# A fused attention kernel on one core: the order of masked copies, reciprocals and value products in its first stage

## The reference

```python
# batch 4, heads 8, seq 576, head_dim 64; window = 128
scores = (q @ k.T) / 8 + slope[h] * -(i - j)
scores = where((i - j >= 0) & (i - j < window), scores, -1e9)
attn = exp(scores - max); attn /= attn.sum(-1) + 1e-9
x = (attn @ v)                       # heads side by side: batch x 576 x 512
h = relu(x @ w_in)                   # 512 -> 1024, halves u and v
v_s = w_spatial @ layernorm(v) + b_spatial
x = (u * v_s) @ w_out
# then: gate, top 2 of 4 experts, causal attention per expert, sum
```

## Time and profile before

| | us |
|---|---|
| three runs: median (lowest to highest) | 489.86 (488.61 to 491.36) |
| the profiled execution | 489.27 |
| its span, from the first to the last instruction | 487.4 |
| busy in it: TensorE / its weight loads | 475.3 / 408.5 |
| busy in it: VectorE / ScalarE / GpSimd | 317.8 / 272.9 / 202.9 |

### The profile page before, as it was taken

The page is one execution under the profiler, slowest core; times in us unless marked ns, Lnnn a source line. Parts: engine busy times, 40 slices in busy tenths (PEclk is TensorE's granted clock), DMA queues, the critical chain, the costliest instruction groups (busy, mean ns, idle before and its releaser), DMA issues.

```text
span 487.4 us, 10761 instructions
## 1 busy us (share of the span) xinstructions
PE 475.3 (98%) x3858; PEld 408.5 (84%) x3858; DVE 317.8 (65%) x1247; ACT 272.9 (56%) x827; POOL 202.9 (42%) x373
## 2 busy tenths in 40 slices
PE   8799999999999999999999999999999999999996
PEld 5577998999776789999876689999877679999974
DVE  7886775367778855337778855436777875235783
ACT  6776572346676644245766745334776663335663
POOL 4361614523434418742244525760343443461431
PEclk9899999999999999999999999999999999999999
DMA  7919420004110081002311073002301000000111
GB/s 230 326 64 245 179 86 1 1 1 135 46 33 23 13 240 42 1 0 53 107 34 44 1 196 98 1 1 48 101 32 56 0 1 2 2 1 12 38 45 54
DMA packets 33512, 31.64 MB, mean 65 GB/s; under 512 B 6002, under 2 KB 24434, under 8 KB 33460
## 3 DMA queue, kind: packets, MB, share of 16 engines
q1 hardware_dynamic: 33460, 30.97, 21.2%
HBM read 23.88 MB, written 4.72 MB: 59 GB/s over the span
## 4 chain that ended last, share of the span: by engine, by line
PE 66%; DVE 17%; ACT 11%; issue 4%; POOL 1%; DVEq 0%
PE bank L1412 14%; PE bank L1414 14%; PE bank L1413 14%; ACT p L830 7%; PE bank L1399 5%; PE bank L1483 5%; DVE ring L943 4%; PE bank L1441 3%; DVE p L1194 2%; PE bank L1690 2%; PE bank L1668 2%; PE bank L1418 2%; DVE ring L954 2%; PE bank L1419 1%; DVE pt L1030 1%
## 5 line engine op out<-in xcount | busy, mean ns | idle before, releaser
L539 POOL TENSOR_SCALAR ring<-ring,r 128x128 f32<-128x128 f32 x144 | 60.2, 430 | 86.1 <-DVE r L963 85.8
L625 POOL TENSOR_SCALAR p<-p,r,wgt 128x128 f32<-128x128 f32 (+3 forms) x64 | 38.3, 610 | 93.3 <-DVE wgt_last L1241 50.0
L653 ACT ACTIVATE ring<-ring,neg 128x128 f32<-128x128 f32 x144 | 56.7, 396 | 21.3 <-DVE ring L954 18.1
L830 ACT ACTIVATE p<-p,neg 128x128 f32<-128x128 f32 (+4 forms) x72 | 41.6, 579 | 29.6 <-DVE neg L1194 29.6
L943 DVE CUSTOM_DVE_ANT_0 ring<-bank,bias 128x256 f32<-128x256 f32 (+1 forms) x128 | 43.5, 384 | 2.3 <-PE bank L1399 2.0
L589 POOL TENSOR_TENSOR g_lo<-uT,g_hi 128x288 fp32r<-128x288 f32 x32 | 25.2, 814 | 36.4 <-ACT g_hi L796 20.4
L1412 PE MATMUL bank<-g_hi,w_c_hi 128*128 128x288 f32 x128 | 38.6, 301 | 0.2
L1412 PE MATMUL bank<-x_hi,w_in_hi 128*128 128x288 f32 x128 | 38.2, 298 | 0.0
L1412 PE MATMUL bank<-w_spatial_hi,vn_hi 128*128 128x288 f32 x128 | 37.8, 295 | 0.0
L1414 PE MATMUL bank<-x_hi,w_in_lo 128*128 128x288 f32 x128 | 37.7, 295 | 0.0
L1414 PE MATMUL bank<-w_spatial_hi,vn_lo 128*128 128x288 f32 x128 | 37.7, 294 | 0.0
(11 more groups left out here) (193 smaller groups left out, 1449.0 us busy)
## 6 DMA issues: line engine op xcount, KB each, us to landing
v_in<-v SPq DMA_DIRECT2D x16, 256.0 KB, 4.0
out<-o_sb SPq DMA_DIRECT2D x16, 256.0 KB, 2.0
q<-qT SPq DMA_DIRECT2D x15, 256.0 KB, 4.6
k<-kT SPq DMA_DIRECT2D x15, 256.0 KB, 5.1
v_minus_v_of_tile_above<-v SPq DMA_DIRECT2D x9, 256.0 KB, 3.8
w_in_raw<-w_in SPq DMA_DIRECT2D x4, 512.0 KB, 6.2
w_cat_raw<-wcat SPq DMA_DIRECT2D x1, 1544.0 KB, 6.8
w_spatial_raw<-wsT SPq DMA_DIRECT2D x1, 1152.0 KB, 9.3
```

The costliest lines, as they stand in the source:

```text
L539: last = nc.gpsimd.tensor_scalar(p, p, r1[:, i % 2, h:h + 1], 0.0, ALU.mult, ALU.add)
L625: nc.gpsimd.tensor_scalar(p, p, r3[:, i % 2, e:e + 1], by, ALU.mult, ALU.mult).then_inc(s3_sd, 1)
L653: nc.scalar.activation(x, x, ACT.Exp, bias=neg1[:, u % SLOTS1:u % SLOTS1 + 1], scale=-1.0, accum_out=sum1[:, i % 2, h:h + 1]).then_inc(s1_ ...
L830: nc.scalar.activation(p, p, ACT.Exp, bias=neg3[:, w % 4:w % 4 + 1], scale=-1.0, accum_out=sum3[:, i % 2, es[0]:es[0] + 1]).then_inc(s3_ex, 1)
```

## The change

Four orders change; no instruction is added or taken away.

On TensorE, `values1(m)` issues the unmasked products of both groups, then waits for the masked copy, then issues the masked products of both. Before, it waited for the masked copy between the first group's unmasked and masked products. Since the two groups' sums are now open at once in one bank, only the first group of a tile (g % 4 == 0) starts with the flag that clears the bank.

On ScalarE, at m = 3 and 5 `copy_pt1(m)` goes ahead of both exponentials instead of between them, so that the copy of m = 3 lies between group 8 and group 9. In row 0 the splitting of `w_in` parts (1, 0) and (1, 1) goes ahead of the exponentials of group 8.

On VectorE, at m = 3 the masked copy goes from behind `join1(10)` and `reciprocal1(9)` to ahead of them, at m = 5 from behind `reciprocal1(13)` and `join1(14)` to directly behind `bias1(14)`; at m = 2 `reciprocal1(6)` and `reciprocal1(7)` each move ahead of the bias step they stood behind, at m = 0 `reciprocal1(3)` moves ahead of `join1(5)`, at m = 5 `join1(14)` moves ahead of `reciprocal1(13)`. In row 0 `low_w_in(1, 0)` and `(1, 1)` go ahead of `join1(9)`.

```diff
@@ ScalarE, row @@
                     elif m == 2:
                         copy_pt1(2)
-                        for g in (6, 7, 8):
-                            exp1(b, g)
+                        exp1(b, 6)
+                        exp1(b, 7)
+                        if first:
+                            high_w_in(1, 0)
+                            high_w_in(1, 1)
+                        exp1(b, 8)
+                    elif m in (3, 5):
+                        copy_pt1(m)
+                        exp1(b, 2 * m + 3)
+                        exp1(b, 2 * m + 4)
...
-                            if first and at[k] == m:
+                            if first and at[k] == m and m != 2:
                                 high_w_in(half, k)
@@ VectorE, row @@
                     if m == 0 and not first:
                         copy_pt1_second(0)
+                        reciprocal1(b, 3)
                         join1(b, 5)
-                        reciprocal1(b, 3)
                         reciprocal1(b, 4)
...
                     elif m == 2:
                         copy_pt1_second(2)
                         join1(b, 7)
+                        reciprocal1(b, 6)
                         bias1(b, 8)
-                        reciprocal1(b, 6)
+                        reciprocal1(b, 7)
                         bias1(b, 9)
-                        reciprocal1(b, 7)
                         join1(b, 8)
+                        if first:
+                            low_w_in(1, 0)
+                            low_w_in(1, 1)
                         join1(b, 9)
+                    elif m == 3:
+                        bias1(b, 10)
+                        reciprocal1(b, 8)
+                        copy_pt1_second(3)
+                        join1(b, 10)
+                        reciprocal1(b, 9)
+                        bias1(b, 11)
+                        join1(b, 11)
+                        reciprocal1(b, 10)
+                    elif m == 5:
+                        bias1(b, 14)
+                        copy_pt1_second(5)
+                        join1(b, 14)
+                        reciprocal1(b, 13)
+                        bias1(b, 15)
+                        join1(b, 15)
+                        reciprocal1(b, 14)
                     elif m < ND1 - 3:
                         bias1(b, 2 * m + 4)
-                        if m == 3:
-                            reciprocal1(b, 8)
-                        else:
-                            reciprocal1(b, 2 * m + 3)
+                        reciprocal1(b, 2 * m + 3)
                         join1(b, 2 * m + 4)
-                        if m == 3:
-                            reciprocal1(b, 9)
                         copy_pt1_second(m)
...
@@ TensorE, values1 @@
-                                                    values[:, h, :], pt[:, part, c:c + r], start=start, stop=stop)
+                                                    values[:, h, :], pt[:, part, c:c + r], start=start, stop=stop,
+                                                    skip_group_check=qb > 0)
...
                     for g in (2 * m, 2 * m + 1):
-                        product(g, v_in[:, qb - 1], 0, True, False)
-                        if g % 2 == 0:
-                            pe.wait_ge(s1_h2, ND1 * b + m + 1)
+                        product(g, v_in[:, qb - 1], 0, g % 4 == 0, False)
+                    pe.wait_ge(s1_h2, ND1 * b + m + 1)
+                    for g in (2 * m, 2 * m + 1):
                         if first:
                             product(g, v_in[:, qb], 1, False, False)
                         product(g, v_step[:, qb - 1], 1, False, True)
```

2 lines of the change are left out of this document (1 added, 1 removed).

## The result

The changed kernel takes 485.39 us, the median of seven runs (484.71 to 486.76); the kernel before, run beside it, 489.38 us (median of seven, 488.59 to 491.36). The ratio is 0.9925, with a 95% interval from 0.9903 to 0.9946: 0.75% faster. The profiled execution of the changed kernel is the quickest of its seven, 484.71 us with a span of 482.9 us, against 489.27 and 487.4 before.

What follows compares the result with a forecast made beforehand. TensorE, busy 98% of the span, bounds the kernel; only its first-stage waits can be won. 3.0 us for rows 1 to 3 plus 1.4 for row 0 gives 4.4, so 485.2 us, range 482.3 to 488.6.

Steps and rivals of the forecast that it cites:

- m = 0: Rows 1 to 3, group 3's reciprocal ahead of a join: rescale starts earlier, 0.2 us a row taken (bounds 0 and 0.33).
- m = 2 and 3: Rows 1 to 3: waits ahead of group 7's transposes and m = 3's masked products go; next scores 0.85 us earlier.
- what is late next?: Question asked at m = 2 and 3 once group 7's wait goes; answer: ScalarE, group 8's exponentials, whose join comes 0.2 us later.
- m = 5: Rows 1 to 3: masked copy is there before TensorE's masked products, so their wait goes, 0.33 us a row.
- The give-backs of `low_x`: Rows 1 to 3: `low_x(1)` and `low_x(2)` each end some 0.2 us after TensorE wants them, subtracted twice a row.
- Row 0: First batch row: earlier `w_in` splits start TensorE's products sooner, part lost waiting for m = 4's masked copy; 1.4 us taken.
- The reordered products: TensorE's new value product order costs nothing; bounds 0.05 us either way for each of 32 masked steps, 1.6 us in all.
- A: Rival: VectorE and ScalarE set the pace from m = 3 to 5; a row keeps 0.4 us, 487.5 us; chance 0.20 with D.
- B: Rival: rescales of groups 8 and 9 drawn out, m = 4's transposes wait 2.4 us; 492.4 us, slower; chance 0.08.
- C: Rival: no new `low_x` wait, 1.7 us a row, 2.4 in row 0; 481.8 us; within the forecast's 0.72 chance.
- D: Rival: transposes, not exponentials, hold m = 3's copy, so moving it wins nothing in rows 1 to 3; chance 0.20 with A.

Runs made afterwards that it cites:

- the corrected kernels: Changed kernel with bias 15 ahead of reciprocal 13 and the masked copy reading PSUM: 484.18 us; with row 0's `low_x(1)` behind m = 4's masked copy too: 483.62 us.

## Why the prediction was right, and where it wasn't

The forecast was 485.2 us, the measurement 485.39. The sum held, 3.0 for rows 1 to 3 against 2.76 measured and 1.4 for row 0 against 1.54. Step by step it was less right than that, and some of the closeness is luck. The schedule was that of row 1, which gained 0.81; three such rows make 2.4, and the other 0.3 is row 2's longer wait, which the schedule didn't know. And the forecast counts from 489.86 and 489.27 us, while the kernel before came out at 489.38 in seven runs: between the medians the gain is 3.99, not 4.4.

**m = 0: right.** 0.2 taken, 0.26 by the run that undoes it, and the wait that it removes is 0.24.

**m = 2 and 3: right in mechanism, 0.07 too large.** The scores of m = 4 start 1.02 us earlier against the transposes of m = 0 (13.21 instead of 14.23), where the steps say 0.2 + 0.85. With 0.24 of that from m = 0, 0.78 is left for m = 2 and 3. That the reciprocals alone would only move the wait to the copy was the reading of "what is late next?", and the run with them alone shows it: 0.76 us removed, nothing won. Alone m = 2 gives -0.08 a row, and taking m = 3 away costs 0.63. That the two need each other is argued from these; the changed kernel without the reciprocals' order of m = 2 wasn't run. What the working had too low was the masked copy, 0.69 us where 0.83 were needed, since the rescale of group 8 now runs beside it. That leaves the wait of some 0.18 us ahead of the masked products of m = 3 that was forecast to go, and of which reading PSUM takes 0.14. I had let only GpSimd suffer from that meeting; VectorE does as well. The rescale itself, 1.40 us, was allowed for and within its slack.

**m = 5: wrong.** I credited 0.33 us, because the wait for the masked copy goes. It goes, and in rows 1 and 3 the step is worth nothing: undone, the stretches are 0.05 us shorter. Only row 2 gains by it, 0.27 us. The step that failed is the question "what is late next?" for TensorE at this place. I followed the copy, the rescale of group 13 and `low_x(2)`, but not the scores of m = 8, which wait for bias 15. On VectorE that step stands behind the masked copy, join 14 and reciprocal 13 in either order, so the edit only changes which of two waits of TensorE takes the time; and it had 0.05 us of slack, as the rows above show. One look at the slack of the next instruction with a reader would have given 0.05 in place of 0.33. And the wait takes back more than the 0.33: the gap ahead of these scores grew from 0.17 to 0.66 us, by 0.49. TensorE was early by 1.02 and by 0.33, but from the transposes of m = 0 the last reading of bias 15 comes only 0.78 us earlier (21.44 instead of 22.22), and with the 0.05 of slack that is the 0.83 by which the scores of m = 8 come earlier (21.64 instead of 22.47). So the row's gain is what VectorE's chain gained, and not a sum over TensorE's waits.

**The give-backs of `low_x`: wrong.** Twice 0.2 us were taken off for `low_x(1)` and `low_x(2)`. Neither wait is there. `low_x(1)` starts at 157.20, 1.59 us after the scores of m = 4 where the working had 1.7, and it's there by 157.89, in time for the `v_product` at 157.95. The working's own figures gave a wait of 0.1 there, and I had rounded it up to 0.2; the rest is the 0.1 us by which it comes earlier after the scores than worked out. `low_x(2)` has time because the scores of m = 8 are late: it ends at 165.56, and its `v_product` stands at 165.90 without a gap. The errors are of opposite sign: m = 5 with the scores behind it gave 0.33 - 0.49 where 0.33 was credited, and 0.4 too much was taken off for `low_x`. So the row's sum of 1.0 came out near the 0.81 by luck in these terms.

**Row 0: right in size, and the clock right for the changed kernel.** The first `v_product` was forecast at 19.3 and stands at 18.84, the masked copy of m = 3 at 20.96 and stands at 20.55, the scores at 22.7 and stand at 22.32; all three are 0.4 to 0.5 early, 0.27 of it the earlier start of this execution. The wait for the masked copy of m = 4 is there at 27.56, and the stretch's gain is 1.54, where 1.55 was worked out for full clock and 1.4 taken. It's a gain over an execution at half clock; at full clock 1.26 of it are the early splits. What wasn't asked is how the order of m = 3 acts in row 0: it costs 0.29 there.

**The reordered products: the cost of zero was right, their worth was booked elsewhere.** By the traces they win 0.5 us alone in three rows, with the new queues 1.0 in all. The bound of 1.6 us either way wasn't needed.

**The rivals.** A, that VectorE and ScalarE set the pace and TensorE's earlier arrival lengthens its waits: right in mechanism, wrong in price. They set it now as far as the scores of m = 8, and TensorE waits 0.49 us longer there, though for a bias step and not for `low_x`. But before, their chain passed through TensorE at m = 3 and 4, so it got shorter too, and 0.8 a row came through and not 0.4. B, the drawn-out rescales: they appear (1.40 and 1.34 us) and cost 0.14 a row through the masked copy, not 1.5. C, all waits gone: the corrected kernels are on the way to it, 1.2 a row of the 1.7. D, that the transposes hold the copy of m = 3: they don't, it starts at 153.47, right behind the exponentials of group 8 (the second at 153.09), while the transposes end at 153.16. The order of m = 3 without the reciprocals of m = 2 wasn't run; the reciprocals alone are at 489.34.

**What is still open: the clock of the kernel before.** Its profiled execution had a granted clock of 0.67, 0.50, 0.50 and 0.62 in the four microseconds from 20 to 24 (the earlier trace rows shows the second of them). It isn't always so. Of 38 executions of it timed beside the experiments, 24 had a mean granted clock of 0.992 to 0.997 and took 489.55 us in the median, 14 had 0.999 to 1.0 and took 488.53. With the changed kernel and every edit of it the mean granted clock was 0.999 or more in each run. So about 0.9 us of the 4.0 between the medians goes with the clock, and against the kernel before at full clock the change wins 3.1 us. The Trainium skill ("TensorE: Matmul & The Clock Gate", section "Part 1: The HAM clock gate") says that the same kernel can measure differently since the hardware's watch on activity isn't tied to the kernel's start. The two kinds of execution counted above fit that, and no run here shows that it's the cause. The idle time right ahead of `v_product` doesn't decide by itself. With the reciprocals alone TensorE has a gap of 2.28 us there and the clock is 0.55 between 21 and 22 us:

```profile
21.05 0.27 PEld L1412 LDWEIGHTS bank<-w_in_hi,x_hi 128*128 128x128 f32 x1 [2.28 <-issue]
```
```profile
21.00:22.00 1.00, 0.92 (x2) 0.81 (x3) 1.00 (x4) 0.98 (x5) 0.00 (x0) 0.55 1.00 336
```

With the `w_in` order undone the gap is 2.28 us too and the clock 1.00; the mean is 0.999 in all four runs. The time with nothing but transposes doesn't part these two kernels either: from the end of the value products of m = 2 to the first `v_product` it's about 3.4 us in both, as in the kernel before, and 1.9 us in the changed kernel. But with the reciprocals alone the mean clock was 0.997 in only five of ten executions, so the four with the `w_in` order undone are few to say that its clock never falls. That the shorter time without products keeps the clock up in the changed kernel is possible and not shown.

## What to carry to other kernels

A wait removed is a gain only up to the next thing that is late: the largest gap of this stage (0.76 us) gave nothing alone, and a removed gap of 0.33 us came back as one of 0.33 more at the next scores (0.66 against 0.33 without that edit). When instructions of a queue change places, look for the first one behind all of them that somebody waits for, and read its slack: it comes at the sum of the rest, in whatever order they stand, and that slack is all that the exchange can win there. Here that held in two rows of three; the third had a delay of its own that the exchange took away, so look at more rounds than one. And where one order serves all rounds of a loop, look at the first round by itself: here the order that wins 0.63 us in each of three rows costs 0.29 in the one that has extra work in the same queues.

## What the runs showed of the hardware

- GpSimd and VectorE slow each other down, both ways. A rescale pair of 0.72 us takes 1.34 to 1.40 beside a masked copy and a join that read two SBUF tensors each, and the masked copy takes 0.83 instead of 0.69. With one of the copy's inputs in PSUM both go back (0.72 to 0.81, and 0.69), at no cost in the copy itself: 0.69 us from either memory.
- Opening two sums in one bank, with the products of one group between those of the other, costs TensorE nothing that these rows show: sixteen products of m = 4 count 1.02 us in the chain of the kernel with the new product order alone, as in the earlier trace rows.
- A gap of 2.28 us on TensorE was followed by a granted clock of 0.55 in the profiled execution of one kernel and by 1.00 in that of another, as told above; of the first kernel five executions of ten had the lower mean clock (0.997).
